# A routed expert layer's result rows: gathering them per block of tokens, and adding them on GpSimd

## What is computed

```python
logits = x @ w_gate
noise_scale = np.log1p(np.exp(x @ w_noise))
noisy_logits = logits + noise_scale * noise
top2 = np.argpartition(-noisy_logits, 2, axis=1)[:, :2]
...
top2_w = np.exp(top2_l)
top2_w /= top2_w.sum(-1, keepdims=True) + 1e-09
out = np.zeros((N, D), dtype=np.float32)
for e in range(E):
    for k in range(2):
        mask = top2[:, k] == e
        ...
        h = np.maximum(x[mask] @ w1[e], 0.0)
        out[mask] += top2_w[mask, k, None] * (h @ w2[e])
```

## Time and profile before

| | us |
|---|---|
| median of 3 runs | 761.95 (761.75 to 764.86) |
| the profiled execution, its own time | 762.46 |
| its span in the profile | 760.3 |
| first gather of pass 0, of pass 1 on POOL | 689.12, 730.70 |
| last matmul of `down(29)`, first of `down(30)` | 737.78, 745.71 |
| first and last addition on DVE start | 746.0, 753.2 |
| last store of `out` is issued | 755.8 |

### The profile page before, as it was taken

One profiled execution on the slowest core, in us unless ns is written; L12 is line 12 of the kernel. 1 busy time (PEld: TensorE's weight loads), 2 busy tenths in 40 slices (PEclk: granted clock), 3 DMA queues, 4 the chain that ended last, 5 costly groups with the idle time before them and its releaser, 6 DMA issues.

```text
span 760.3 us, 12845 instructions
## 1 busy us (share of the span) xinstructions
PE 734.4 (97%) x3884; PEld 617.0 (81%) x3885; DVE 361.7 (48%) x879; ACT 229.2 (30%) x528; POOL 437.1 (57%) x240
## 2 busy tenths in 40 slices
PE   7999999999999999999999999999999999999983
PEld 6677898999889988999877788888888878888762
DVE  4777543234423432453474554454454544544526
ACT  5999622223223322332321221121121112212200
POOL 6888997000300030018969968677887889923562
PEclk8999999999999999999999999999999999999996
DMA  8642484000200020006453867577867777746658
GB/s 279 256 141 94 146 297 174 0 1 1 84 1 0 0 83 0 0 28 235 159 215 101 287 207 262 190 238 248 246 225 255 244 245 248 242 146 207 211 170 283
DMA packets 60221, 122.49 MB, mean 161 GB/s; under 512 B 7072, under 2 KB 22048, under 8 KB 60192
## 3 DMA queue, kind: packets, MB, share of 16 engines
q1 hardware_dynamic: 28512, 63.92, 25.0%
q10 hardware_dynamic: 27840, 45.62, 18.1%
q0 software_dynamic: 3840, 12.59, 4.7%
HBM read 82.26 MB, written 39.85 MB: 161 GB/s over the span
## 4 chain that ended last, share of the span: by engine, by line
PE 85%; DMA 7%; DVE 2%; POOL 2%; ACT 1%; issue 1%; SPq 0%; ACTq 0%; DVEq 0%; POOLq 0%
PE bank L1547 19%; PE bank L1454 18%; PE bank L1404 18%; PE bank L1576 18%; DMA ring_raw<-in_moe_w 5%; PE bank L1357 4%; PE bank L1348 3%; PE bank L1330 3%; PE bank L1529 2%; DMA hid_lanes<-hid_by_lane 1%; PE bank L1470 1%; DVE gathered_a L1314 1%; PE bank L1464 1%; POOL ring L641 1%; ACT arena L744 1%
## 5 line engine op out<-in xcount | busy, mean ns | idle before, releaser
L1576 PE MATMUL bank<-ring,hidT_hi 128*128 (+1 forms) x496 | 159.5, 402 | 10.2 <-DVE hidT_lo L1179 10.2
L641 POOL TENSOR_TENSOR ring<-ring_raw,ring 128x2048 fp32r<-128x2048 f32 x32 | 148.2, 4632 | 2.5
L687 POOL DMA_INDIRECT sorted_x<-y_rows,arena x24 | 25.2, 1051 | 204.4 <-DVEq L1102 198.3
L639 POOL TENSOR_TENSOR ring<-ring_raw,ones 128x2048 fp32r<-128x2048 f32 x32 | 115.9, 3622 | 44.6 <-DMA ring_raw<-in_moe_w 44.4
L1547 PE MATMUL bank<-ring,xsT_hi 128*128 (+1 forms) x496 | 133.4, 391 | 3.3 <-DVE hid L1166 2.1
L1454 PE MATMUL bank<-w_out_sb,gated_hi 128*128 128x512 f32 x384 | 121.1, 397 | 0.0
L1576 PEld LDWEIGHTS bank<-ring,hidT_hi 128*128 128x128 f32 x496 | 91.6, 190 | 31.3 <-issue 11.2
L1547 PEld LDWEIGHTS bank<-ring,xsT_hi 128*128 128x128 f32 x496 | 92.6, 188 | 24.0 <-issue 4.7
L1576 PE MATMUL bank<-ring,hidT_lo 128*128 (+1 forms) x248 | 98.3, 396 | 0.0
L1023 DVE TENSOR_TENSOR arena<-bank,arena 128x384 f32<-128x384 f32 x64 | 35.6, 557 | 115.2 <-ACT arena L799 114.2
L1404 PE MATMUL bank<-xT_hi,w_in_hi 128*128 (+1 forms) x256 | 86.7, 339 | 0.0
(11 more groups left out here) (185 smaller groups left out, 1011.5 us busy)
## 6 DMA issues: line engine op xcount, KB each, us to landing
ring_raw<-in_moe_w SPq DMA_DIRECT2D x48, 512.0 KB, 4.4
hid_by_lane<-hid ACTq DMA_DIRECT2D x29, 512.0 KB, 3.5
hid_lanes<-hid_by_lane ACTq DMA_DIRECT2D x29, 512.0 KB, 4.4
ring_raw<-in_moe_w SPq DMA_DIRECT2D x8, 1024.0 KB, 6.4
sorted_y<-ys ACTq DMA_DIRECT2D x31, 256.0 KB, 2.2
xs<-sorted_x ACTq DMA_DIRECT2D x27, 256.0 KB, 3.7
sorted_y<-zeros SPq DMA_DIRECT2D x1, 4864.0 KB, 25.1
arena<-in_k SPq DMA_DIRECT2D x8, 520.0 KB, 4.0
```

The lines of the kernel that those rows point to most:

```text
L639: pool.tensor_tensor(hi, raw, one_like(raw), ALU.mult).then_inc(rounded, 1)
L641: ins = pool.tensor_tensor(lo, raw, hi.bitcast(F32), ALU.subtract)
L1576: last = pe.matmul(bank[5][:, :], x[:, c * P:(c + 1) * P], ring[:, bass.ds(at * 2 * WE + (w + CH * FE + c * DM), DM)], start=c == 0 and n ...
```

## The change

**POOL.** Both passes now go block by block. `stores_i` becomes a table of 4 blocks by 2 passes: in pass kk, block blk waits for the tiles up to the end of the expert before the last but one (kk = 0) or the last (kk = 1), and for as many tiles of that expert as hold the rows that blocks 0 to blk have placed in it. DVE works this table out from `placed`, a copy of `carry` per block, in nine small instructions ahead of its loop. As soon as group i is being gathered, POOL finishes group i - 2: a multiplication in pass 0 (`scale`), a multiplication and an addition in pass 1 (`combine`). DVE's 12 additions are gone. `gathered_a` and `gathered_b` swap places, since `gathered_a` is now filled while the weights in that half of the ring are still read.

**The last tiles.** `hidT_hi` and `hidT_lo` get a second pair and `down` a second bank (6), used by tiles 28 and 30. `up(29)`, `down(27)` and the steps around them leave the loop, and tile 30's hidden rows are transposed by PE inside `down(29)`, in front of its last three chunks, with no DMA.

```diff
-        gathered_b = place_at("gathered_b", X_HI, [TT, DM])
+        gathered_a = place_at("gathered_a", X_HI, [TT, DM])
...
-        gathered_a = place_at("gathered_a", RING_AT + (E % RING) * 2 * WE, [TT, DM])
+        gathered_b = place_at("gathered_b", RING_AT + (E % RING) * 2 * WE, [TT, DM])
...
+            def gather(kk, rows, i):
+                if i >= 2 + kk:
+                    pool.wait_ge(gathered[kk][i - 2 - kk], 16)
+                pool.indirect_dma_start(
...
+            def scale(i):
+                pool.wait_ge(gathered[0][i], 16)
+                pool.tensor_tensor(gathered_a[:, i, :], gathered_a[:, i, :],
+                                   gate_at[0][:, i:i + 1].to_broadcast([P, DM]), ALU.mult).then_inc(scaled, 1)
+            def combine(i):
+                pool.wait_ge(gathered[1][i], 16)
+                pool.tensor_tensor(gathered_b[:, i, :], gathered_b[:, i, :],
+                                   gate_at[1][:, i:i + 1].to_broadcast([P, DM]), ALU.mult).then_inc(scaled, 1)
+                pool.wait_ge(scaled, TT + i + 1)
+                pool.tensor_tensor(gathered_a[:, i, :], gathered_a[:, i, :], gathered_b[:, i, :],
+                                   ALU.add).then_inc(summed, 1)
...
+            pool.wait_ge(gates_ready, 2)
+            for kk, rows, finish in ((0, gathered_a, scale), (1, gathered_b, combine)):
+                for blk in range(NBLK):
+                    stores = pool.value_load(stores_i[0:1, blk, kk:kk + 1], min_val=16, max_val=16 * TILES)
+                    pool.wait_ge(scattered, 16 * TOP * TT)
+                    pool.wait_ge(ys_stored, stores)
+                    for i in range(blk * KB, blk * KB + KB):
+                        gather(kk, rows, i)
+                        if i >= 2:
+                            finish(i - 2)
+                for i in range(TT - 2, TT):
+                    finish(i)
...
             with act.Fori(4, TILES - 2) as t:
                 tile(t)
-            tile(TILES - 2, load=False)
+            relu_out(TILES - 2)
+            hid_out(TILES - 2)
+            rows_turned_out(TILES - 1)
+            hid_turned_out(TILES - 3, b=1)
+            store_rows(TILES - 4)
+            hid_in(TILES - 2)
             store_rows(TILES - 3)
-            hid_turned_out(TILES - 2, used=TILES - 1)
+            hid_turned_out(TILES - 2, used=TILES - 2)
             relu_out(TILES - 1)
-            hid_out(TILES - 1)
-            hid_in(TILES - 1)
-            hid_turned_out(TILES - 1, used=TILES)
+            hid_turned_out(TILES - 1, used=TILES - 1, b=1)
             store_rows(TILES - 2)
...
+                dve.tensor_copy(placed[:, bass.ds(blk, 1), :].rearrange("p b e -> p (b e)"), carry[:, KB, :])
...
+            link(dve.tensor_tensor(placed_swap[:, :, :], placed[:, :, :],
+                                   swap[:, None, :].to_broadcast([P, NBLK, E]), ALU.mult))
...
+            link(dve.tensor_tensor(placed_end[:, :, :], placed_tiles[:, :, :],
+                                   tile_end_t[:, None, E - TOP - 1:E - 1].to_broadcast([P, NBLK, TOP]), ALU.add))
+            dve.tensor_scalar(stores_i[:, :, :], placed_end[:, :, :], 16.0, None, ALU.mult).then_inc(stores_known, 1)
...
-            with dve.Fori(4, TILES - 1) as t:
+            with dve.Fori(4, TILES - 2) as t:
                 tile(t)
+            relu_out(TILES - 2, written=True)
+            rows_turned_out(TILES - 1)
+            turn_hidden(TILES - 3)
+            hid_turned_out(TILES - 3, 1)
+            result_out(TILES - 4)
+            result_out(TILES - 3, b=1)
             turn_hidden(TILES - 2)
-            result_out(TILES - 3)
             hid_turned_out(TILES - 2)
             relu_out(TILES - 1, written=True)
-            turn_hidden(TILES - 1)
+            hid_turned_out(TILES - 1, 1)
             result_out(TILES - 2)
-            hid_turned_out(TILES - 1)
-
-            for i in range(TT):
-                dve.wait_ge(gathered[1][i], 16)
-                dve.wait_ge(scaled, i + 1)
-                dve.scalar_tensor_tensor(gathered_a[:, i, :], gathered_b[:, i, :], gate_at[1][:, i:i + 1],
-                                         gathered_a[:, i, :], ALU.mult, ALU.add).then_inc(summed, 1)
...
-            with pe.Fori(4, TILES - 1) as t:
+            with pe.Fori(4, TILES - 2) as t:
                 up(t, evicted=True)
                 turn_rows(t + 1)
                 down(t - 2)
-            down(TILES - 3)
+            up(TILES - 2, evicted=True)
+            turn_rows(TILES - 1)
+            down(TILES - 4)
+            down(TILES - 3, b=1, evicted=TILES - 4)
             up(TILES - 1, evicted=True)
-            down(TILES - 2)
-            down(TILES - 1)
+            down(TILES - 2, evicted=TILES - 3, turned=TILES - 1)
+            down(TILES - 1, b=1, evicted=TILES - 2)
```

More of the change, by code:

```diff
@@ L231, in build @@
         ranks = part([TT, E])
+        placed = part([NBLK, E])
         chosen_all = [part([TT, E]) for k in range(TOP)]
@@ L262, in build @@
         tile_end_i = part([E], I32)
-        stores_i = part([2], I32)
+        stores_i = part([NBLK, TOP], I32)
+        placed_swap = part([NBLK, E])
+        placed_d = part([NBLK])
+        placed_tiles = part([NBLK, TOP])
+        placed_end = part([NBLK, TOP])
         filled = part([E])
@@ L335, in build @@
         part([FE])
+        hidT_hi.append(place_at("hidT_hi_last", ARENA + used[0], [FE], F32R))
+        part([FE])
+        hidT_lo.append(place_at("hidT_lo_last", xsT_at + 2 * DM, [FE], F32R))
+        assert FE == 2 * DM
         hid_cols = hid[:, :].rearrange("p (r c) -> p c r", c=EC)
@@ L389, in build @@
         gates_ready = sem("gates_ready")
+        slots_known = sem("slots_known")
         stores_known = sem("stores_known")
@@ new lines, in gather @@
+            def gather(kk, rows, i):
+                if i >= 2 + kk:
+                    pool.wait_ge(gathered[kk][i - 2 - kk], 16)
+                pool.indirect_dma_start(
+                    out=rows[:, i, :], out_offset=None, in_=sorted_y[:, :],
+                    in_offset=bass.IndirectOffsetOnAxis(ap=ordered[kk][:, i:i + 1], axis=0),
+                ).then_inc(gathered[kk][i], 16)
+            def scale(i):
+                pool.wait_ge(gathered[0][i], 16)
+                pool.tensor_tensor(gathered_a[:, i, :], gathered_a[:, i, :],
+                                   gate_at[0][:, i:i + 1].to_broadcast([P, DM]), ALU.mult).then_inc(scaled, 1)
@@ L885, in hid_turned_out @@
                     act.wait_ge(hid_turned, 2 * t + half + 1)
-                    act.copy(hidT_hi[:, half * BANK:(half + 1) * BANK], bank[3 + half][:, :]).then_inc(hidT_rounded, 1)
+                    act.copy(hidT_hi[b][:, half * BANK:(half + 1) * BANK], bank[3 + half][:, :]).then_inc(hidT_rounded, 1)
             def store_rows(t):
@@ L921, in _, with tile @@
             hid_in(3)
-            def tile(t, load=True):
+            def tile(t):
                 relu_out(t)
@@ L945, in _ @@
             act.wait_ge(ys_stored, 16 * (TILES - 1))
-            act.copy(ys[:, :], bank[5][:, :]).then_inc(ys_ready, 1)
+            act.copy(ys[:, :], bank[6][:, :]).then_inc(ys_ready, 1)
             store_rows(TILES - 1)
@@ L1178, in hid_turned_out @@
                     dve.wait_ge(hidT_rounded, 2 * t + half + 1)
-                    dve.tensor_tensor(hidT_lo[:, cols], bank[3 + half][:, :], hidT_hi[:, cols].bitcast(F32),
+                    dve.tensor_tensor(hidT_lo[b][:, cols], bank[3 + half][:, :], hidT_hi[b][:, cols].bitcast(F32),
                                       ALU.subtract).then_inc(hidT_ready, 1)
@@ L1559, in turn_hidden, with down @@
                     last.then_inc(hid_turned, 1)
-            def down(t, first=False, known=False, rows=None):
+            def down(t, first=False, known=False, rows=None, b=0, evicted=None, turned=None):
                 e = 0 if known else pe.value_load(tile_expert_i[0:1, bass.ds(t, 1)], min_val=0, max_val=E - 1)
@@ L1574, in down @@
                         turn_rows(rows)
-                    for n, (x, w) in enumerate(((hidT_hi, 0), (hidT_hi, WE), (hidT_lo, 0))):
-                        last = pe.matmul(bank[5][:, :], x[:, c * P:(c + 1) * P],
+                    if turned is not None and c == EC - 3:
+                        turn_hidden(turned)
+                    for n, (x, w) in enumerate(((hidT_hi[b], 0), (hidT_hi[b], WE), (hidT_lo[b], 0))):
+                        last = pe.matmul(bank[5 + b][:, :], x[:, c * P:(c + 1) * P],
                                          ring[:, bass.ds(at * 2 * WE + (w + CH * FE + c * DM), DM)],
```

50 lines of the change are left out of this document (21 added, 29 removed).

## The result

| | median us (range, runs) | ratio to before, with its 95% interval |
|---|---|---|
| before | 763.26 (761.58 to 765.43, 20) | |
| changed | 767.15 (761.57 to 772.66, 20) | 1.0052 [1.0028, 1.0077] |

Slower by 0.5%, where 0.8% faster was forecast, and the runs of the changed kernel spread over 11 us instead of 4. The profiled execution took 771.69 us with a span of 769.9: 9.6 us more than the 760.3 of before. It is one of the long ones.

What follows compares the result with a forecast made beforehand. PE, busy 97% of the span, was taken as the bound, with a queue of POOL, DVE and SP at the end. Span 753.8 + 0.1 + 2.16 outside it gave 756.1, forecast as 756.0 us, range 753.0 to 761.0.

Steps and rivals of the forecast that it cites:

- Small things on DVE: Ahead of DVE's loop: nine small operations take 1.9 us, cost 0; the copy of `placed` costs 0 to 0.15 us.
- Rival B: Last part, pass 1: neighbours stretch POOL's multiplication and addition pairs by 0.73 us each, 5.8 in all, giving 761.8; chance 0.14.
- The thresholds: Pass 1 on POOL: stores of tiles 25 to 28 open the four blocks, the first three at 700.5, 712.0, 723.3 us.
- D: Start of pass 1: thresholds don't open early, POOL starts the whole pass at 730, time 780 us; chance 0.03.
- POOL's chain: End of pass 1: from tile 27's store POOL is busy without a gap from 723.3 for 27.1 us, to 750.4.
- PE: Tiles 28 to 30: no new stall, low clock gone, `down(30)` ends at 743.1; the 10 us gain is limited by POOL.
- E: Tiles 22 to 27: slow DMA landings starve PE before tile 27, giving about 762 to 766 us; chance 0.06.
- the sum of 756.1: Whole kernel: span 753.8 plus 0.1 for a copy and 2.16 outside the span, 6.4 us less than the profiled execution.
- The version with the additions on DVE: End of the kernel: POOL only gathers, tile 30's store decides; span 746.6 to 749.0, time about 750 us.

Runs made afterwards that it cites:

- x1_fixed: The changed kernel with operands of its nine small DVE instructions moved to PSUM (ten instructions with the extra copy): 759.65 us, ratio 0.9939.
- x3: The kernel before plus the copy of `carry` and the small DVE instructions with operands in PSUM, result unused: 763.98 us, ratio 1.0008.
- y1_moved: The changed kernel with its nine small DVE instructions unaltered but moved earlier, to where POOL issues scatters: 762.27 us, ratio 0.9973.
- y3_pool_only: The kernel before with only POOL's part of the change, operands in PSUM, last tiles as before: 759.99 us, ratio 0.9946.
- y2_tail_only: The kernel before with only the change of the last tiles; POOL's passes and DVE's additions as before: 759.86 us, ratio 0.9940.

## Why the prediction failed, point by point

- **The step that failed** is "Small things on DVE": nine dependent small operations "about 0.2 us each, 1.9 us", after which `relu_out(4)` comes "some 0.5 us later", at a cost of 0. Measured: 11.9 us on DVE, of which 10.7 in three instructions, a stall of 8.45 us and 2.9 us of low clock in the profiled execution; between the changed kernel and x1_fixed 3.6 us in the lowest runs, 7.5 in the medians, 12.5 in the highest. That the place takes 2 us for nothing was right (x3). The step also looked at `relu_out(4)` alone, while the stalled `up(5)` waited for `xsT_lo`, which DVE writes behind it. What was wrong is a duration taken from instructions of like size with other operands and another neighbour: the step asked how many elements, not where they lie and what POOL does meanwhile.
- **Rival B had the mechanism and the wrong victim.** It asked whether DVE would stretch POOL, and only in the last 60 us. The 1.69 us that it took as the highest price of an addition was such a meeting, the one at 115.42 us above, and that "no run here shows it yet" was wrong: the 13 long `gated_lo` do. The Trainium skill, GPSIMD Engine Reference, key points, which it cited, names DVE instructions with two SBUF inputs and those in a two-port mode. L1334 and L1337 are of the first kind. L1345, a `tensor_scalar` from SBUF to SBUF, would be of the second; no row here shows its mode. The Trainium skill, SBUF — State Buffer, section on the two separate sides, goes further: whichever of the two engines starts first keeps the pair of SBUF ports that they share for its whole instruction, and the other is blocked. The end times of DVE's held small instructions and POOL's agree with it within 0.07 us in four profiled executions. With it, or with the 13 rows of `gated_lo`, at hand, the row of `split` (up to 4.6 us) and not the row of a small instruction would have been the upper bound for each of the three.
- **The thresholds** opened where they were counted (D falls): pass 1 starts at 716.3 as soon as pass 0 is through (705.9 in x1_fixed, for 700.5 forecast, which cost nothing as block 2 decides), and its next blocks at 727.3 and 739.7 behind the stores of tiles 26 and 27.
- **POOL's chain** was 25.9 us (739.73 to 765.66) for a forecast of 27.1: multiplication 1.05, addition 1.29 as taken, and nearly no gap between. From tile 27's store to the first gather it was 4.35 us for 2.9, and from the last addition to the end of the span 4.2 for 3.4. The store then has 3.6 us in its way, not 2.2.
- **PE** waits for no engine and runs at full clock from 670 us to the end of `down(27)` (E falls), and behind it too, as forecast.
- **The forecast of the rest.** x1_fixed is the change as the prediction imagined it: 759.65 for 756.0. Its profiled execution took 758.17, 2.1 more than the sum of 756.1: block 2 starts at 726.18 instead of 723.3 (the dip, and 3.74 us behind the store), POOL needs 1.1 us less, the last landing takes 0.8 more, which gives the span of 756.4 for 753.8. That sum was right in kind, 2.1 us short of this execution and 3.7 of the median.
- **The version with the additions on DVE** was put at "about 750": 751.10.

## What to carry to other kernels

Before you put a small instruction on VectorE, look at its operands and at what GpSimd does then: here one with two inputs in SBUF, or the scalar operation from SBUF to SBUF, lasted until the end of the operation on tensors that GpSimd was in, however small it was itself; one input in PSUM, or a place in the order where GpSimd only issues DMAs, freed it. Look first in the trace that you have for instructions with the same kind of operands that are sometimes longer than their median. A wider spread of the runs is a weak sign: the changed kernel's went over 11 us, but y1_moved and y3_pool_only, with none of the small ones held, went over 7.2 and 6.3. And of two changes to the end of a kernel, cost each against the end that the other leaves: here 4 us and 4 us made 4.5.

## What was not expected of the hardware

- An instruction of 8 elements per partition takes 4.40 us beside a split of 4.61 us, and 0.17 us with one operand in PSUM. A `TENSOR_REDUCE` from SBUF to SBUF inside POOL's instruction (433.19 in the changed kernel) was not held, at 0.19 us.
- POOL's issues of indirect DMAs don't hold DVE (0.17 to 0.19 us beside scatters, 0.75 us per addition beside gathers), but in y2_tail_only three issues took 1.34 to 1.35 us instead of 0.95, each started 0.23 to 0.24 us after DVE had started to add; the first, behind 738.05:

```profile
738.29 1.34 POOL L737 DMA_INDIRECT gathered_b<-sorted_y,arena  x1 [0.30 <-issue]
```
